# Attention, a mixing layer and routed experts on one core: bias matmuls of the attention placed ahead of the maxima's transposition, zero matmuls in TensorE's first pauses, third pair's queries and keys loaded earlier

## The reference

```python
scores = scale * np.matmul(q, k.transpose(0, 1, 3, 2))
bias = slopes[:, None, None] * (-np.abs(rel).astype(np.float32))[None, :, :]
mask = (rel >= 0) & (rel < window)          # window = 128
scores = np.where(mask, scores + bias[None], -1000000000.0)
scores = scores - np.max(scores, axis=-1, keepdims=True)
attn = np.exp(scores)
attn = attn / (np.sum(attn, axis=-1, keepdims=True) + 1e-09)
return np.matmul(attn, v).astype(np.float32)
```

## Time and profile before

| | us |
|---|---|
| median of 3 runs | 951.38 (951.3 to 951.42) |
| the profiled execution | 951.46 |
| its span, first to last instruction | 949.5 |
| TensorE busy | 877.5 (92%) |
| VectorE, ScalarE, GpSimd busy | 466.8, 309.4, 284.1 |
| attention: first to last transposition (L659) | 16.36 to 158.09 |

### The profile page before, as it was taken

How to read it: one execution, slowest core, us unless ns; L and a number is a source line. 1 busy time by engine, 2 the same in 40 slices (tenths; PEclk the granted TensorE clock), 3 DMA queues, 4 the chain that set the end, 5 groups by cost and what they waited for, 6 DMA issues and landing times.

```text
span 949.5 us, 22638 instructions
## 1 busy us (share of the span) xinstructions
PE 877.5 (92%) x9128; PEld 637.4 (67%) x9129; DVE 466.8 (49%) x843; ACT 309.4 (33%) x425; POOL 284.1 (30%) x298
## 2 busy tenths in 40 slices
PE   5788888899999999999999999975999999999995
PEld 3566666677676767676767676733777777777773
DVE  5889897655533333333333333657995886000000
ACT  3677777443321212121212121220332322333231
POOL 2466776501110101020202010001354444334432
PEclk9999999999999999999999999986999999999998
DMA  8255452506301010101010100521775674111110
GB/s 295 67 160 174 141 160 78 165 23 179 128 23 45 23 44 22 44 22 44 24 42 33 33 22 22 183 63 46 237 240 169 212 229 159 44 41 44 44 32 1
DMA packets 55342, 89.24 MB, mean 94 GB/s; under 512 B 7140, under 2 KB 26035, under 8 KB 55165
## 3 DMA queue, kind: packets, MB, share of 16 engines
q1 hardware_dynamic: 49853, 72.56, 24.3%
q0 software_dynamic: 5440, 16.00, 5.3%
HBM read 71.19 MB, written 16.55 MB: 92 GB/s over the span
## 4 chain that ended last, share of the span: by engine, by line
PE 84%; DVE 8%; DMA 3%; issue 2%; ACT 1%; POOL 1%; DVEq 0%; SPq 0%; POOLq 0%; ACTq 0%
PE psum L827 20%; PE psum L844 20%; PE psum L1000 13%; PE psum L1016 13%; PE psum L619 5%; PE psum L778 3%; PE psum L766 2%; DVE m_mem L1285 2%; DVE arena L1313 2%; PE psum L967 1%; PE psum L644 1%; PE psum L675 1%; PE psum L788 1%; DVE m_mem L1289 1%; DVE m_mem L1299 1%
## 5 line engine op out<-in xcount | busy, mean ns | idle before, releaser
L827 PE MATMUL psum<-m_mem,arena 128*128 (+1 forms) x1728 | 198.8, 273 | 0.3 <-DVE arena L1547 0.3
L844 PE MATMUL psum<-arena,m_mem 128*128 128x512 f16 x864 | 195.3, 379 | 0.0
L827 PEld LDWEIGHTS psum<-m_mem,arena 128*128 128x128 f16 x1728 | 168.4, 98 | 26.0 <-DVE arena L1547 0.6
L844 PEld LDWEIGHTS psum<-arena,m_mem 128*128 128x128 f16 x864 | 84.5, 98 | 90.4
L1000 PEld LDWEIGHTS psum<-m_mem,arena 128*128 x2400 | 137.3, 97 | 7.0 <-issue 1.5
L1000 PE MATMUL psum<-m_mem,arena 128*128 128x128 f16 x2400 | 139.7, 219 | 1.2 <-issue 0.6
L1016 PE MATMUL psum<-arena,m_mem 128*128 x600 | 133.4, 379 | 0.0
L1156 ACT ACTIVATE m_mem<-psum 128x512 f16<-128x512 f32 x72 | 42.9, 596 | 246.4 <-PE psum L827 245.9
L1016 PEld LDWEIGHTS psum<-arena,m_mem 128*128 128x128 f16 x600 | 57.6, 98 | 65.2
L1792 POOL TENSOR_TENSOR arena<-m_mem,arena 128x1024 f16<-128x1024 f32 x9 | 18.0, 1998 | 270.8 <-ACT arena L1171 225.8
L1455 DVE SCALAR_TENSOR_TENSOR m_mem<-psum,m_mem 128x512 f16<-128x512 f32 x72 | 49.7, 690 | 99.7 <-ACT m_mem L1156 99.5
(11 more groups left out here) (217 smaller groups left out, 1086.6 us busy)
## 6 DMA issues: line engine op xcount, KB each, us to landing
dimdft_sb<-in_exp_w SPq DMA_DIRECT2D x74, 256.0 KB
wstage<-in_exp_w SPq DMA_DIRECT2D x54, 256.0 KB
m_mem<-in_qk SPq DMA_DIRECT2D x16, 576.0 KB, 4.5
arena<-in_v SPq DMA_DIRECT2D x32, 160.0 KB, 4.3
x_rows<-m_mem SPq DMA_DIRECT2D x16, 320.0 KB, 3.4
x_rows<-arena SPq DMA_DIRECT2D x9, 512.0 KB, 2.8
wstage<-in_mlp_w SPq DMA_DIRECT2D x16, 256.0 KB
arena<-in_mlp_w SPq DMA_DIRECT2D x16, 256.0 KB, 3.3
```

What stands on the lines that cost most here:

```text
L827: last = nc.tensor.matmul(psum[:, 2 + k % 4, (f % 2) * 2 * P:(f % 2 + 1) * 2 * P], w1_sb[:, sp_, c, f * P:(f + 1) * P], unT[:, bass.ds(t % ...
L844: last = nc.tensor.matmul(psum[:, 6 + q, :], hT[:, k % 4, sp_, at:at + P], w2_sb[:, mp, f, :], start=f == 0 and sp_ == 0 and mp == 0, stop ...
```

## The change

- `first_bias(p)`: the bias of the first scores is its own function, issued for pair p + 1 just ahead of the transposition for pair p. It waits for the third maximum of pair p. `scores(p, 0)` is now the products alone.
- `bias_t(p, u)`: the bias of the transposed scores is its own function. For u = 0 it starts the accumulation and is issued ahead of `first_bias` and the transposition; for u = 1 it stays at the head of its block.
- The transposed row goes to spare columns of bank 7, where banks 6 and 7 also hold the results of `pv`. `normalise` therefore also waits for `row_copied` of the pair in hand. The wait for the copied row moves from ahead of the first products of `scores_t(p, 0)` to ahead of its `less_max`.
- `warm(n)`: n matmuls of zeros (64 weight columns, 512 moving columns, from `qk_pads`, which VectorE clears early) into bank 6: 14 at the very start, 4, 4 and 3 behind the three scores of pair 0, and 4 and 4 in the first iteration where later ones have `pv`.
- SP loads queries and keys of pair 2, with its wait for the first split, ahead of the weight blocks and tables.

The terms that are summed stay the same; their order changes.

The diff, cut to its core:

```diff
--- before.py
+++ after.py
@@ -87,6 +87,8 @@
 RING = 2 + SPARE
 MID = TOK // 2
 ONES = 20
+PADS_SET = 15
+ROW_AT = 384
 
 
 QS = 16.0
@@ -497,6 +499,8 @@
             for p in range(2):
                 for a in range(2):
                     load_v(p, a)
+            sp.wait_ge(qk_lo, 1)
+            load_qk(2, 0)
             for n in range(4):
                 load_w(n)
             sp.dma_start(ident_sb[:, :], ident).then_inc(const_in, 16)
@@ -523,8 +527,6 @@
                 sp.dma_start(eo[0:REST, p % 3, 4], x16[0:REST, p % 2, 2]).then_inc(xsh_in[p % 2], 16)
                 sp.dma_start(eo[REST:TAIL, p % 3, 4], x16[REST:TAIL, p % 2, 4]).then_inc(xsh_in[p % 2], 16)
 
-            sp.wait_ge(qk_lo, 1)
-            load_qk(2, 0)
             for p in range(PAIRS):
                 if p + 3 < PAIRS:
                     sp.wait_ge(qk_lo, p + 2)
@@ -623,65 +625,67 @@
 
             def scores(p, j):
 
-                if j == 0:
-                    pe.wait_ge(qk_lo, p + 1)
-                if j > 0 or p > 0:
-                    pe.wait_ge(max_done[j - 1], p + (1 if j > 0 else 0))
+                if j > 0:
+                    pe.wait_ge(max_done[j - 1], p + 1)
                 def units(last):
                     for t, col in SUNITS[j]:
                         done = products(p, 0, (col, col + SKEYS[t]), 0, t * P, 1, SKEY0[t], j > 0 and col == 0,
                                         last and t == SUNITS[j][1][0])
                     return done
 
-                if j > 0:
-                    units(False)
+                if j == 0:
+                    pe.wait_ge(qk_lo, p + 1)
+                    units(True).then_inc(scores_ready[0], 1)
+                    return
+                units(False)
                 for a in range(2):
                     table = bias_sb[:, p % PPB * 2 + a, :]
-                    if j == 0:
-                        nc.tensor.matmul(psum[:, a, 0:P], biasid_sb, table[:, P:2 * P], start=True, stop=False)
-                        nc.tensor.matmul(psum[:, a, P:3 * P], biasid_sb, table, start=False, stop=False)
-                    elif j == 1:
+                    if j == 1:
                         last = nc.tensor.matmul(psum[:, a, :].rearrange("p (t k) -> p t k", t=2), biasid_sb,
                                                 twice(table), start=False, stop=True)
                     else:
                         last = nc.tensor.matmul(psum[:, a, 0:P + TAIL], biasid_sb, table[:, 0:P + TAIL],
                                                 start=False, stop=True)
-                if j == 0:
-                    last = units(True)
                 last.then_inc(scores_ready[j], 1)
 
-            row_bank = psum[:, 2, 0:P // 2].bitcast(BF16)
+            def first_bias(p):
+
+                if p > 0:
+                    pe.wait_ge(max_done[2], p)
+                for a in range(2):
+                    table = bias_sb[:, p % PPB * 2 + a, :]
+                    nc.tensor.matmul(psum[:, a, 0:P], biasid_sb, table[:, P:2 * P], start=True, stop=False)
+                    nc.tensor.matmul(psum[:, a, P:3 * P], biasid_sb, table, start=False, stop=False)
+
+
+            row_bank = psum[:, 7, ROW_AT:ROW_AT + P // 2].bitcast(BF16)
 
             def max_to_row(p):
                 pe.wait_ge(neg_ready, p + 1)
-                if p > 0:
-                    pe.wait_ge(p_lo[0], p)
                 nc.tensor.transpose(row_bank, neg_parts.rearrange("p h n -> p (h n)"), identh_sb)\
                     .then_inc(row_ready, 1)
 
+            def bias_t(p, u):
+
+                if p > 0:
+                    pe.wait_ge(p_lo[u], p)
+                for a in range(2):
+                    table = bias_sb[:, p % PPB * 2 + a, :]
+                    same, behind = table[:, P:2 * P], table[:, 0:P]
+                    o = psum[:, 2 + 2 * u + a, :].rearrange("p (n q) -> p n q", n=2)
+                    nc.tensor.matmul(o[:, :, 0:P], same, twice(biasid_sb), start=True, stop=False)
+                    if u == 0:
+                        nc.tensor.matmul(o[:, :, P:2 * P], behind, twice(biasid_sb), start=False, stop=False)
+                    else:
+                        nc.tensor.matmul(o[:, 1, P:2 * P], behind, biasid_sb, start=False, stop=False)
+                        nc.tensor.matmul(o[:, 0, P:P + TAIL], behind, biasid_sb[:, 0:TAIL], start=False, stop=False)
+                        nc.tensor.matmul(o[:, 0, P + TAIL:2 * P], same, biasid_sb[:, 0:TAIL], start=False, stop=False)
+
             def scores_t(p, u):
 
-                if u == 0:
-                    pe.wait_ge(row_copied, p + 1)
-                if p > 0 and u == 1:
-                    pe.wait_ge(p_lo[u], p)
                 at = 2 + 2 * u
 
...
-                def less_max(last):
+                def less_max():
                     for t in ((0, 1, 2), (2, 3, 4))[u]:
                         for a in range(2):
...
-                            done = nc.tensor.matmul(o, rowsel_sb[rows, t, :], m, start=False, stop=last and t == 4)
+                            done = nc.tensor.matmul(o, rowsel_sb[rows, t, :], m, start=False, stop=t == 2 + 2 * u)
                     return done
 
-                if u == 1:
-                    bias(True, False)
                 for c in ((0, 1), (2, 3, 4))[u]:
                     col = CPLACE[c][1]
-                    products(p, at, (col, col + CQUERIES[c]), 1, c * P, 0, c * P, c == 0)
-                last = less_max(u == 1)
+                    products(p, at, (col, col + CQUERIES[c]), 1, c * P, 0, c * P, False)
                 if u == 0:
-                    last = bias(False, True)
-                last.then_inc(st_ready[u], 1)
+                    pe.wait_ge(row_copied, p + 1)
+                less_max().then_inc(st_ready[u], 1)
 
             def pv(p, a):
                 if a == 0:
@@ -727,31 +728,54 @@
                 if a == 1:
                     last.then_inc(pv_done, 1)
 
+            def warm(n):
+
+                for _ in range(n):
+                    nc.tensor.matmul(psum[0:TAIL, 6, :].rearrange("p (a b) -> p a b", b=TAIL), qk_pads[:, 0, :],
+                                     qk_pads[:, 0, :].unsqueeze(1).to_broadcast([P, 512 // TAIL, TAIL]), start=True, stop=True)
+
+            pe.wait_ge(ones_set, PADS_SET)
+            warm(14)
             pe.wait_ge(ones_set, ONES)
             pe.wait_ge(att_in, 2 * 16)
-            for j in range(3):
+            def turn(p):
+
+                if p + 1 < PAIRS:
+                    if p == 0:
+                        pe.wait_ge(bias_in, 16)
+                    first_bias(p + 1)
+                max_to_row(p)
+
+            first_bias(0)
+            for j, n in enumerate((4, 4, 3)):
                 scores(0, j)
-            max_to_row(0)
+                warm(n)
+            bias_t(0, 0)
+            turn(0)
             for p in range(PAIRS):
                 more = p + 1 < PAIRS
-                if p == 0:
-                    pe.wait_ge(bias_in, 16)
                 if more:
                     scores(p + 1, 0)
                 if p == 0:
                     pe.wait_ge(rowsel_made, 3)
-                for u in range(2):
-                    scores_t(p, u)
+                scores_t(p, 0)
+                bias_t(p, 1)
+                scores_t(p, 1)
                 if more:
                     scores(p + 1, 1)
                 if p > 0:
                     pv(p - 1, 0)
+                else:
+                    warm(4)
                 if more:
                     scores(p + 1, 2)
                 if p > 0:
                     pv(p - 1, 1)
+                else:
+                    warm(4)
                 if more:
-                    max_to_row(p + 1)
+                    bias_t(p + 1, 0)
+                    turn(p + 1)
             def spectrum(b, chunks=range(DC), first=False):
 
                 pe.wait_ge(x_split, PPB * b + PPB)
@@ -1076,7 +1100,7 @@
 
             def copy_row(p):
                 act.wait_ge(row_ready, p + 1)
-                nc.scalar.activation(max_row, psum[:, 2, 0:P // 2].bitcast(BF16), ACT.Copy)\
+                nc.scalar.activation(max_row, psum[:, 7, ROW_AT:ROW_AT + P // 2].bitcast(BF16), ACT.Copy)\
                     .then_inc(row_copied, 1)
 
             def v_hi_of(p, a):
@@ -1316,6 +1340,7 @@
             def normalise(p):
                 o = psum[:, 6:8, 0:ST * (DH + 1)].rearrange("p a (t d) -> p a t d", t=ST)
                 dve.wait_ge(pv_done, p + 1)
+                dve.wait_ge(row_copied, min(p + 3, PAIRS))
                 nc.vector.tensor_scalar(den, o[:, :, :, DH], PS * DEN_EPS, None, ALU.add).then_inc(den_ready, 1)
                 dve.wait_ge(den_ready, p + 1)
                 nc.vector.reciprocal(rden, den).then_inc(rden_ready, 1)
```

13 lines of the change are left out of this document (removed).

## The result

The changed kernel takes **940.52 us** (median of 4 runs, 939.54 to 940.75); the kernel before, measured beside it, 951.34 (4 runs, 950.28 to 951.42). That is 10.8 us faster. The ratio on record is 0.9873, 95% interval 0.9851 to 0.9895; the quotient of the two medians, 0.9886, lies inside it. The forecast of 939.4 us was 1.1 too low.

| | before | predicted | after |
|---|---|---|---|
| T0, first transposition of the maxima | 16.36 | 14.0 | 14.88 |
| T1 | 28.16 | 22.9 | 24.23 |
| T2 | 38.55 | 31.15 | 32.33 |
| mean of the 13 periods to T15 | 9.195 | 8.9 | 8.928 |
| T15 | 158.09 | | 148.40 |

A forecast was written before the change was run, and what follows sets the result against it. It took a circle of waits between TensorE and VectorE, neither full, to set the attention's period. Gains of 7.4 us (start), 3.8 (loop) and 0.8 (last pair) sum to 12.0, giving 939.4 us; range 931.0 to 945.5.

The forecast's parts named there:

- The loop, 3.8 us: 13 steady periods: biases moved into TensorE's idle time cut the period from 9.195 to 8.9 us, saving 3.8 us.
- The floor of 8.28: Steady loop: the shortest period, 4.55 + 3.73 = 8.28 us, if the tiny pair escapes GpSimd.
- The 3.73: Steady loop: VectorE's part from the start of the large maximum to the next transposition, 3.73 us.
- the 4.55: Steady loop: the earliest start of the large maximum after the transposition that VectorE's own queue allows, 4.55 us.
- The start to T2, 7.4 us: Start: raised clock, shorter legs and earlier third-pair load bring T2 from 38.55 to 31.15, saving 7.4 us.
- The early load: Start: third pair's load, moved ahead, lands near 12, at worst 15.7; ScalarE, which sat idle 3.93 us, wants it at 14.5.
- The last pair, 0.8 us: Last pair: its 0.37 us wait for the copied row and its 0.43 us bias go, saving 0.8 us.
- The zeros raise the clock: Start: zero matmuls lift TensorE to the upper clock level; rival that they don't: sum 6.6, 944.9 us, chance 0.12.
- GpSimd holds the period: Loop rival: VectorE and GpSimd wait each other out, period 9.17, no loop gain, 942.9 us; chance 0.15.
- the circle through v: Loop, within the GpSimd rival: the circle of waits through v grows by up to 0.6 us.
- The full gain: Loop rival: the tiny pair escapes GpSimd's instruction, period 8.28, sum 20.1, 931.3 us; chance 0.15.
- Slower: Loop rival: late transfers delay ScalarE's row copy and `normalise` waits; at period 10, 953.6 us; chance 0.03.

The follow-up runs named there:

- e9: The changed kernel with VectorE's tiny pair ahead of the transposition (cast and remainder) written as three reductions: 934.33 us.
- e6: The changed kernel with the load of v for pair p + 4 issued ahead of the moves and the store of pair p: 941.04 us.
- e13: The changed kernel with only the first block of 14 zero matmuls, none of the later ones: 940.84 us.
- e2: The changed kernel with the third pair's queries and keys loaded behind the tables again: 947.85 us.
- e10: The changed kernel with the three reductions, and v of pair p+4 and queries and keys of pair p+5 loaded ahead of the store of pair p: 938.09 us.

## Why the prediction was right, point by point

The sum said 12.0 us; the medians gave 10.8 and the spans 11.1.

- *The loop, 3.8 us.* Measured 3.5, period 8.928 against 8.9. The mechanism is the one argued: TensorE's leg shortened by the moved biases, VectorE's L1309 directly behind L1330, part of it given back because the tiny pair meets GpSimd's instructions more squarely. e9 shows the last part by taking it away. That the mean came within 0.03 is partly luck. By the sum the cast waits for the first of two L1729 and the subtraction for the second; one period of the 13 went so (9.03 us, cast at 48.16). The sum also counted L1301's own 0.17 twice: in the row at 101.66 it ended 0.02 behind L1704, and with that P is 8.79. More details were off: I had every period at 8.87, with the pair at 0.5 to 0.8 each beside L1704's successor; they scatter from 8.16 to 9.99; in 5 of the 13 it is L1735, not L1729, that holds the cast, in 4 the cast alone waits for the second L1729, in one the subtraction alone, in one they wait for L1744 and L1745, in one for nothing.
- *The floor of 8.28.* It was no bound: the period of 8.16 lies under it. Two errors met. The 3.73 still held 0.28 of waiting, since L1299 took 0.45 in that row and takes 0.17 free; with neither of the pair held this part is 3.44. And the 4.55 came out at 4.75, as the split starts at T + 3.28 and not 3.20 and L1309 another 0.11 behind its end. Free of holds the changed kernel would make 8.19; the hold of the pair, 0.72 in the mean, makes up most of the way to 8.93. e9, with three instructions, makes 4.75 + 3.66 = 8.41.
- *The start to T2, 7.4 us.* Measured 6.2, the term of the sum that was most mis-sized. (1) I let the zero block end between 6.7 and 7.5; it ended at 7.65 and the first products started at 8.03, not 7.25. The 14 took 6.18 us here, 5.75 in e6 and 4.79 in e13: by these durations the clock rises at different places in the block from run to run. In e13, with products at 7.02, T0 is 14.36. (2) In T0 to T1 I gave the two `add_row` 1.67 us, as before; they took 1.94, and products that I put at T0 + 1.5 started at T0 + 1.85. L1309 came at T0 + 5.68, not 5.2, and T1 - T0 was 9.35, not 8.9. T1 to T2 was 8.10 against 8.25.
- *The early load.* ScalarE's wait of 3.93 us is gone, and the fourth pair's load, the tightest cover, was in time (no wait at 24.65). e2 shows what it is worth.
- *The last pair, 0.8 us.* T15 to the end shrank by 1.4. Its products follow the transposition with no wait for the copied row, as argued; the other 0.6 I can't place, as this part lay between 789.5 and 792.3 us over all kernels run.
- *The zeros raise the clock.* The rival (0.12) that zeros alone don't is out: with them 0.67 and 0.83 us, without 1.14 and 1.46 for the same products. The sign named for it, 0.66 us per 12 of 256 columns, was too low: 0.83 with the drain, and the row of 0.67 has 128 columns in half of its matmuls.
- *GpSimd holds the period* (0.15), 942.9 us. Its special step, that L1306 (now L1330) and L1700 (now L1725) wait each other out, is half right. The split was not held by an L1725 in flight (1.36 at 79.45, first L1725 from 78.71), but the second L1725, which starts during it, was: the two take 2.97 us at 78.71 instead of 2.10. The period stayed at 8.93 and not 9.17, so the circle through v did not close; why is not shown, though GpSimd had waited 2.84 us for v just before. The rival also took the cast L1299 as a case of the rule for two SBUF inputs; it has one, so of the two tiny instructions only L1301 bears on that rule. It is e6 and e10 that come near this rival, with another instruction of GpSimd.
- *The full gain* (0.15): not here, since the pair does not escape. *Slower* (0.03): ScalarE's copy of the row was never late; it starts 0.3 us behind each transposition, and `normalise` never waited.

## What to carry to other kernels

Two short instructions on the path can cost more than the long ones beside them: a cast of ten numbers a partition took up to 1.43 us where GpSimd was busy, and writing it and its remainder as reductions gave 6 us, as much as the move of eight matmuls a pair had given alone. A transfer that comes "late" may be what keeps two engines apart in time; pulling it forward (e10) is then a loss, so after each change look again at what stands beside what. A result of no change (e6) can be two changes that cancel; the two parts of the period show it. And parts of a start-up are not to be priced one by one: the early load was worth 3.1 us without the zeros and about 7 with them.

## What was not expected of the hardware

- Matmuls whose operands are all zeros raise TensorE's clock as others do: the block of 14 takes 4.8 to 6.2 us, and what follows it runs at the upper level (2.4 GHz).
- GpSimd's instructions do not all hold VectorE's split of two SBUF inputs. A running L1748 (two inputs) held it nearly until its end (2.43 us at 96.55 in e10, against 1.35); a running L1725 (one input in SBUF) did not (1.35 to 1.44 us in the changed kernel). In the other direction the split did hold L1725, by 0.87 us at 78.71. The Trainium skill ("SBUF — State Buffer", section "Who interferes with whom") has a VectorE instruction with two SBUF inputs contend with a GpSimd instruction that reads SBUF; the trace agrees for L1748 and disagrees for L1725 in flight, and the measurement decides.
- In e13 the granted clock fell to 0.63 between 12 and 16 us and was back at the upper level for the products at 16.44, with no cost that shows in T2 (32.01, 32.33 in the changed kernel).
